# A fused attention and expert kernel on one core: identity transposes ahead of the first products, later casts, stores in pieces, two tiles reordered

## The reference

```python
scores = q @ k.T / sqrt(64)          # block-causal mask, blocks of 64
attn   = exp(scores - max); attn /= attn.sum() + 1e-9
x      = (attn @ v) as [2304, 512]
p      = domain_probs / (sum + 1e-9)               # 4 experts
y      = sum over e of p[:, e] * (relu(x @ w1[e]) @ w2[e])     # 512 -> 1024 -> 512
h      = y @ w_in                                  # 512 -> 1024
solu   = h * softmax(h)
out    = layernorm(solu) * g_ln @ w_out            # 1024 -> 512
```

## Time and profile before

| | |
|---|---|
| median of 3 runs | 1168.68 us (1168.49 to 1169.01) |
| profiled execution, its own time | 1172.1 us |
| its span, first to last instruction | 1170.3 us |
| PE busy | 1140.5 us, 97% |
| DVE, ACT, POOL busy | 55%, 36%, 36% |
| mean granted clock of PE | 0.995 |

### The profile page before, as it was taken

How to read it: one execution, slowest core, us unless ns; L and a number is a source line. 1 busy time by engine, 2 the same in 40 slices (tenths; PEclk the granted TensorE clock), 3 DMA queues, 4 the chain that set the end, 5 groups by cost and what they waited for, 6 DMA issues and landing times.

```text
span 1170.3 us, 16702 instructions
## 1 busy us (share of the span) xinstructions
PE 1140.5 (97%) x6114; PEld 1020.3 (87%) x6114; DVE 645.2 (55%) x1155; ACT 425.8 (36%) x927; POOL 415.7 (36%) x403
## 2 busy tenths in 40 slices
PE   7999998899999999999999999999999999999998
PEld 6999888888989999999999999999999977888886
DVE  7999987554244534333444334452434468667774
ACT  6888876231223311112321112321112344433432
POOL 6898886572434200005400004410002463433320
PEclk8999999999999999999999999999999999999999
DMA  4575765985563313071504052512225100000000
GB/s 140 184 223 177 233 224 182 366 288 207 194 219 117 127 57 132 9 252 55 207 1 189 1 195 85 186 57 103 87 82 198 37 18 10 27 20 27 19 27 36
DMA packets 67477, 146.28 MB, mean 125 GB/s; under 512 B 5968, under 2 KB 34640, under 8 KB 67280
## 3 DMA queue, kind: packets, MB, share of 16 engines
q1 hardware_dynamic: 67408, 145.36, 35.6%
HBM read 114.60 MB, written 30.74 MB: 124 GB/s over the span
## 4 chain that ended last, share of the span: by engine, by line
PE 79%; DVE 5%; POOL 5%; DMA 4%; issue 3%; ACT 2%; SPq 1%; DVEq 0%; POOLq 0%; ACTq 0%
PE s L1700 34%; PE outp L1564 18%; PE s L1564 12%; PE ring L1564 10%; DMA work<-x_rows 2%; PE ring L1575 1%; DVE neg_max L1179 1%; PE ring L1831 1%; POOL x_late L749 1%; ACT pr L894 1%; DVE ptr_l L1186 1%; PE outp L1610 1%; PE outp L1609 1%; DVE k_l L1191 1%; DMA xr<-x_stash 1%
## 5 line engine op out<-in xcount | busy, mean ns | idle before, releaser
L1700 PE MATMUL s<-xr,w1s 128*128 128x384 f32 x2016 | 360.4, 337 | 4.8 <-DVE u L1394 4.3
L1700 PEld LDWEIGHTS s<-xr,w1s 128*128 128x128 f32 x2016 | 351.8, 188 | 9.5 <-DVE u L1394 5.0
L1034 ACT ACTIVATE hid_h<-u 128x384 fp32r<-128x384 f32 x96 | 50.4, 525 | 365.5 <-DVE u L1389 338.7
L708 POOL TENSOR_TENSOR work<-work 128x256 f32<-128x256 f32 x20 | 15.9, 796 | 395.2 <-DMA work<-in_moe_w 269.3
L1344 DVE SCALAR_TENSOR_TENSOR hid_l<-s,hid_h 128x384 fp32r<-128x384 f32 x48 | 26.8, 557 | 124.8 <-ACT hid_h L1030 124.8
L1564 PE MATMUL s<-k_h,qb 128*128 128x288 f32 (+8 forms) x320 | 78.1, 332 | 10.1 <-DVE qb L1262 5.6
L1700 PE MATMUL s<-w1s,yop_h 128*128 128x512 f32 x252 | 85.7, 399 | 1.9 <-POOL yop_l L851 0.7
L1301 DVE TENSOR_TENSOR u<-s,m_b 128x384 f32<-128x384 f32 x24 | 13.4, 558 | 130.0 <-PE s L1700 130.0
L1030 ACT ACTIVATE hid_h<-s 128x384 fp32r<-128x384 f32 x48 | 23.6, 491 | 157.6 <-PE s L1564 154.5
L894 ACT ACTIVATE pr<-s,neg_max 128x576 f32<-128x576 f32 (+2 forms) x144 | 75.6, 533 | 6.8 <-DVE neg_max L1179 6.5
L1564 PE MATMUL outp<-w_h,hid_h 128*128 128x512 f32 x192 | 75.5, 393 | 0.0
(11 more groups left out here) (170 smaller groups left out, 2454.0 us busy)
## 6 DMA issues: line engine op xcount, KB each, us to landing
xr<-x_stash SPq DMA_DIRECT2D x77, 768.0 KB, 6.4
r_sb<-r_scratch SPq DMA_DIRECT2D x16, 576.0 KB, 4.3
x_rows<-x_n SPq DMA_DIRECT2D x32, 288.0 KB, 4.7
work<-x_rows SPq DMA_DIRECT2D x24, 384.0 KB, 6.5
x_stash<-x_tmp SPq DMA_DIRECT2D x12, 768.0 KB, 4.2
work<-in_moe_w SPq DMA_DIRECT2D x32, 256.0 KB, 3.9
stage<-in_moe_w SPq DMA_DIRECT2D x32, 256.0 KB, 4.9
x_stash<-xr SPq DMA_DIRECT2D x1, 5376.0 KB, 21.6
```

What stands on the lines that cost most here:

```text
L708: pool.tensor_tensor(s1, a21, a22, ALU.add).then_inc(w1_sums, 1)
L1034: act.activation(hid[slot][0][:, :], source, ACT.Relu).then_inc(hid_high, 1)
L1700: last = pe.matmul(target, x, y, start=start and i == 0, stop=stop and i == 2, skip_group_check=True)
```

## The change

PE makes 17 transposes of the identity into `ring` as soon as the identity exists, which POOL now makes first. POOL starts on the queries of pair 1 only when DVE has split those of pair 0. DVE makes `key_low(1)` behind all row maxima of pair 0. In the steps 10 to 14 the casts and low parts of x, and the load of its second half, are placed otherwise. In `last_step` the product m2 moves ahead of the last turn. The store of `xr` becomes seven stores, issued behind the store of the last pair's output and the loads that follow it. The casts of rounds 0 and 1 with t = 1 move from the middle of units 2 and 6 to their end. In the last stage, `ln_low_part` of the last tile but one goes ahead of the last tile's variance, and the first half of that tile's output ahead of the last `turn_ln`.

```diff
@@ SP
-            def load_x(sg, t):
+            def load_x(sg, t, parts=(0, 1)):
                 for i in range(2):
                     sp.wait_ge(x_stored[i], 16 * min(PAIRS, DC * (sg + 2)))
                 if sg == 0 and t == 0:
                     sp.wait_ge(w1_ready, 3 * HALF_F)
+                elif parts == (1,):
+                    sp.wait_ge(x_added, 2 * sg + t)
                 elif 2 * sg + t < 3:
                     sp.wait_ge(x_low, NR * (2 * sg + t - 1) + 2)
...
                 if n == 1:
-                    sp.wait_ge(stash_stored, 16)
+                    sp.wait_ge(stash_stored, 16 * NP)
...
                 if p == 9:
                     load_x(0, 0)
+                if p == 12:
+                    load_x(0, 1, (0,))
                 if p + 2 < PAIRS:
                     load_k(p + 2)
                 store_r(p)
                 spread_r(p)
-                if p == 12:
-                    load_x(0, 1)
+                if p == 11:
+                    load_x(0, 1, (1,))
...
-            sp.wait_ge(x_low, 2 * NR)
-            sp.dma_start(x_stash[0, :, :], xr[:, :].bitcast(f32)).then_inc(stash_stored, 16)
+            def stash_first(slots):
+                for i in slots:
+                    at = i * SLOT
+                    sp.dma_start(x_stash[0, :, at:at + SLOT], xr[:, at:at + SLOT].bitcast(f32)).then_inc(stash_stored, 16)
+
             store_x(PAIRS - 1)
-
             sp.wait_ge(w2_ready, 2)
             load2(w2[0, :, :], 2)
             load_x(1, 1)
+            sp.wait_ge(x_low, 2 * NR)
+            stash_first(range(0, 3))
             stash_round(1, 0, 0)
             stash_round(1, 0, 1)
             sp.wait_ge(w2_ready, 4)
             load2(w2[0, :, :], 3)
+            stash_first(range(3, NP))
             stash_round(1, 0, 2)
             stash_round(1, 0, 3)
             load_x(2, 0)
@@ POOL
-            pool.memset(v_nat[:, (KC - 1) * P:KC * P], 0.0).then_inc(tail_clear, 1)
             pool.memset(ident[:, :], 0.0).then_inc(consts_step, 1)
             pool.wait_ge(consts_step, 1)
             pool.affine_select(out=ident[:, :], in_=ident[:, :], compare_op=ALU.not_equal, fill=1.0, base=0,
-                               pattern=[[-1, P]], channel_multiplier=1).then_inc(consts_made, 1)
+                               pattern=[[-1, P]], channel_multiplier=1).then_inc(ident_made, 1)
+            pool.memset(v_nat[:, (KC - 1) * P:KC * P], 0.0).then_inc(tail_clear, 1)
...
-            pool.wait_ge(consts_made, 3)
+            pool.wait_ge(ident_made, 1)
+            pool.wait_ge(tail_clear, 1)
+            pool.wait_ge(first_split, 3)
             split_query(1)
             for p in range(PAIRS):
-                if p == 11:
-                    x_low_part(0, 0, 0)
-                if p == 12:
-                    x_low_part(0, 0, 2)
-                    x_low_part(0, 0, 3)
                 split_values(p)
...
                 if p == 11:
+                    x_low_part(0, 0, 0)
                     x_low_part(0, 0, 1)
                 if p == 12:
                     x_join(0, 1)
                 if p == 13:
+                    x_low_part(0, 0, 2)
+                    x_low_part(0, 0, 3)
                     x_add(0, 1, 0)
                     x_add(0, 1, 1)
+                if p == 14:
                     x_low_part(0, 1, 0)
-                if p == 14:
                     x_low_part(0, 1, 1)
@@ ACT
                 if p in (10, 11):
-                    x_cast(0, 0, 2 * (p - 10))
-                if p in (13, 14):
-                    x_cast(0, 1, 2 * (p - 13))
+                    x_cast(0, 0, p - 10)
+                if p == 14:
+                    x_cast(0, 1, 1)
+
+            def nearly_late(p):
+                if p == 11:
+                    x_cast(0, 0, 2)
+                if p == 14:
+                    x_cast(0, 1, 2)
 
             def late(p):
...
-                if p in (10, 11):
-                    x_cast(0, 0, 2 * (p - 10) + 1)
+                if p == 11:
+                    x_cast(0, 0, 3)
                 if p in (13, 14):
-                    x_cast(0, 1, 2 * (p - 13) + 1)
+                    x_cast(0, 1, 3 * (p - 13))
...
                 high(T452, p, par)
+                nearly_late(p)
                 exp_scores(5, n)
...
-                if e == 0 and sg < 2 and u in (1, 2):
-                    x_cast(sg + 1, u - 1, 0)
-                    x_cast(sg + 1, u - 1, 1)
+                if e == 0 and sg < 2 and u == 1:
+                    x_cast(sg + 1, 0, 0)
+                    x_cast(sg + 1, 0, 1)
...
                 hid_rest(m, "c12", 3, u2[:, :])
+                if e == 0 and sg < 2 and u == 2:
+                    x_cast(sg + 1, 1, 0)
+                    x_cast(sg + 1, 1, 1)
@@ DVE
             max_scores(8, 0)
-            max_scores(7, 0)
+            for b in SCORE_ORDER[1:]:
+                max_scores(b, 0)
             key_low(1, 1)
-            for b in SCORE_ORDER[2:]:
-                max_scores(b, 0)
...
             moments(TT - 1)
+            ln_low_part(TT - 2)
             variance(TT - 1)
             normalise(TT - 1)
-            ln_low_part(TT - 2)
             ln_low_part(TT - 1)
@@ PE
                 turn(T452, p, par)
+                up(0, "m2")
                 turn(T0123, p, par)
                 all_right(p)
-                up(0, "m2")
                 up(0, "m7")
...
-            pe.wait_ge(consts_made, 3)
+            pe.wait_ge(ident_made, 1)
+            for _ in range(WARM_TURNS):          # WARM_TURNS = 17
+                pe.transpose(ring[:, 0:P], ident[:, :], ident[:, :])
+            pe.wait_ge(consts_made, 2)
...
             output(TT - 3, 1)
+            output(TT - 2, 0)
             turn_ln(TT - 1)
-            output(TT - 2, 0)
             output(TT - 2, 1)
```

More of the change, by code:

```diff
@@ L54, in build_program @@
     GROUPS_S = len(SCORE_GROUPS)
+    WARM_TURNS = 17
     def keys(b):
@@ L301, in build_program @@
         first_split = sem("first_split")
+        ident_made = sem("ident_made")
         tail_clear = sem("tail_clear")
@@ L540, in load_x @@
                     sp.wait_ge(x_added, 2 * sg + t)
-                for z, rows in enumerate((x_top, x_bottom)):
+                for z in parts:
+                    rows = x_bottom if z else x_top
                     for h in range(2):
```

## The result

The changed kernel takes 1172.91 us (median of 8 runs, 1171.25 to 1173.74), the kernel before beside it 1168.85. The ratio is 1.0031, 95% interval [1.002, 1.0042]. The forecast was 1160.5 us, faster. By the ratio it is slower by some 3.6 us: the sign is wrong, and the value lies outside the range.

The account below looks back on a forecast made before the run. PE's own products were taken as the bound (busy 1140.5 of 1170.3 us), leaving idle and low-clock time to gain. Terms -4.2 - 3.5 - 4.2 + 5.3 - 1.6 = -8.2 off 1168.7 gave 1160.5 us, range 1154.5 to 1166.0.

Parts of the forecast that it names:

- head: Kernel start through attention step 1: transposes, earlier reciprocals and no fall of the clock save 4.2 us; bounds -1.5 and -5.0.
- attention steps 10 to 15: Waits on queries and `ptr_l` go, two casts add 1.6 us to the path: net -3.5 us; bounds -5.0 and -1.0.
- store of the last pair: End of unit 1: PE's 3.34 us stall and 1.3 us of low clock go, 0.4 kept back: -4.2 us.
- casts at the end of units 2 and 6: Copies stall m2 and operands of units 4 and 8 come late: +5.3 us; bounds +1.2 and +9.
- tail: Last stage: PE's 1.69 us wait for a low part goes: -1.6 us; bounds -1.2 and -1.7.
- what is late next, for which 0.4 us had been kept: After the last pair's store: POOL's `x_join` and low parts run beside DVE's combinations, 0.4 us held back.
- slower rival: Four 768 KB `xr` stores delay rounds 2 and 3, stalling unit 2's casts: +11 us, 1171.5 us; chance 0.07.
- The 4.2 us that the prediction set against the rival: Landing time of the stores of rounds 2 and 3, against the over 12 us at which the slower rival decides.
- PE's first wait on `qb`: Kernel start: a sign of the forecast, that this wait is near 1.5 us.
- The rival that the transposes warm nothing: Head: first products stay at the lower clock, so head is -3.0 and the time 1161.7 us; chance 0.2.
- Alone on the queue it should be faster, so I take 1.5 and not 2.1: Unit 8: a 19.5 us chain of casts, low parts, stores and load makes operands late, +1.5 us.
- the third operand: Next group after the casts: PE needs it 17.4 us from the casts, against a 20.6 us chain: +2.6 us.

Follow-up runs that it names:

- e4: The kernel before with only the head's edits (17 transposes, identity first, later query split, `key_low(1)` behind the maxima): 1166.85 us, 0.9994.
- e8: e1 with attention steps 10 to 15 as before the change on all engines: 1166.07 us, 0.9984.
- e1: The changed kernel with the casts of t = 1 back behind c11 in the middle of units 2 and 6: 1163.0 us, 0.9956.
- e10: The kernel before with only SP's new order: last pair's store ahead, store of `xr` in seven pieces: 1170.34 us, 1.0017.
- e2: The kernel before with only the late casts at the end of units 2 and 6: 1175.97 us, 1.0083.
- e9: The kernel before with only the tail's two lines moved: 1166.35 us, 0.9985.
- e5: The kernel before, unchanged, traced in a second execution: 1167.13 us.
- e13: e10 with the last four pieces of the `xr` store moved behind the stores of rounds 2 and 3: 1173.75 us, 1.0049.
- e6: The changed kernel with the casts of units 2 and 6 one place earlier, between ACT's casts of c22 and c21: 1167.88 us, 1.0001.
- e11: e1 with POOL's join for the next super-group behind low parts 2 and 3 of t = 1: 1161.35 us, 0.9947.
- e12: e1 run again, beside e11: 1163.77 us, 0.9963.
- e7: The changed kernel with POOL's join for the next super-group behind two low parts of t = 1: 1172.2 us, 1.0031.
- e3: The changed kernel without its 17 transposes: 1172.15 us, 1.0036.
- e15: e11 with the store of `xr` as before the change, one store ahead of the last pair's: 1160.24 us, 0.9929.
- e14: e11 with the last four pieces of the `xr` store moved behind the stores of rounds 2 and 3: 1165.96 us, 0.9983.

## Why the prediction was wrong

| term | forecast | measured |
|---|---|---|
| head | -4.2 | -0.7 (e4) |
| attention steps 10 to 15 | -3.5 | -3.3 (e8 against e1) |
| store of the last pair | -4.2 | +2.0 (e10) |
| casts at the end of units 2 and 6 | +5.3 | +8.8 (after against e1), +9.7 (e2) |
| tail | -1.6 | -1.8 (e9) |
| sum | -8.2 | +5.0 to +5.9 |

The measured terms are ratios less 1 (or less the other kernel's ratio), times 1168.5 us. Each is uncertain by 1 to 2.5 us, so their sum does not contradict the 3.6 us of the whole. Nor need they add: the +2.0 of the store was measured with early casts, which wait for stores behind the pieces, and the late casts of after do not. An estimate for its place in after is what separates after from e2 (3.1 and 8.3 thousandths, -6.1 us) less head, steps and tail (-5.8): about nothing.

**The store of the last pair, 6 us off.** The term was the stall of 3.34 us and the 1.3 us of low clock. In e5, e2, e9 and e4 the stall is 0.24 to 0.99 us. In e5 ACT did wait too, 6.24 us for the same rows, and PE hardly felt it: most of this wait was slack. The prediction took one execution, itself 3.4 us above the median, and took "the same differences off the median". Where the profiled execution is that far above the median, what it has beyond the others is what a change can't give back. Besides, the pieces are not free. Of what is late next, for which 0.4 us had been kept, PE has the 1.21 us on DVE, in e10 and in after. The slower rival was right that the stores of rounds 2 and 3 are held up by the four pieces, 9.8 us where 4.1 is usual (e10, e5), and right that 12 us decide: in after they had landed when the casts came, so this rival did not come about there. It did in e10, whose casts come earlier, and the whole of the edit costs 2.0 us there. The 4.2 us that the prediction set against the rival is a median over twelve stores of the whole span, and these stand behind 3 MB. The sign of the whole is not explained by this rival.

**The head, 3.5 us off.** By most of its own steps it was right: the transposes fit (1.52 to 5.16), no clock of 0.5 near 16, the gap ahead of step 0 1.30 us, step 1 at 25.84. Only PE's first wait on `qb` is 0.54 us and not 1.5. What failed is the other side of the difference, the head of before. The 1.4 us between steps 0 and 1 were the low spell of one execution: in the five others that have the old head (e5, e2, e9, e10, e13) these steps are 10.7 to 10.8 us apart, after has 10.86, and nothing is gained. Mark 0 is at 15.52, 17.19, 17.36, 15.34 and 17.79 in them, so there the gain is 0.4 to 2.8 us, with 17.33 no rare value. Of this, 0.7 us reach the end in e4. Where the rest goes stays open.

The rival that the transposes warm nothing is refuted (0.73 against 1.16 us for the same products of block 7). The Trainium skill, TensorE: Matmul & The Clock Gate, "Part 4: PE-mode transpose", says that transpose mode does not count as busy for the clock; in after, e6, e11 and e12 the 17 fp32 transposes were all that PE had done when it came to the first product at the higher level, so these traces do not agree. In the other seven with transposes that product still ran at the lower level. Whether the time gains by them is not shown: 1.0031 with them, 1.0036 without.

**The casts, some 4 us off.** The copy of m1 costs 0.97 us twice, forecast 1.1. The wait in unit 2 that was to go, 1.00 in the trace of before, is 0.61 in e1 and gone in after. Unit 4: 3.12 us of waits where e1 has 1.87, and 1.7 us of clock, together 2.9; forecast 2.6. The failed step is unit 8, "Alone on the queue it should be faster, so I take 1.5 and not 2.1". The length of the chain was right in sum: 19.5 us were worked out and 19.4 passed from the casts (305.89) to PE's start on the first load (325.29). Its parts were not, which is luck: 8.4 us to ACT's second cast where 6.6 were forecast, 4.2 from there to the load's issue where 6.6 were, as the load doesn't wait for the last store to land, and 6.8 for the load where 6.3 were. What was wrong is when PE needs it. The prediction asked after the third operand, 17.4 us behind the casts, because the one wait in the trace before stood there. When all seven loads shift together, the first is the late one, and PE wants it at 321.55, 15.7 us behind the casts. 19.4 less 15.7 is the 3.7 us seen. It was the first because SP's written order has all four stores of the round chain ahead of all seven loads, so even the operands of round 1 wait for round 3. The clock that a wait of this size costs, 1.7 us, had been put in the bound and not in the value. By the traces the term is 1.9 less 0.6, and 2.9 and 5.4 (3.74 and 1.7): 9.6 us. This, too, is one execution of after: in the other kernels with late casts the first wait at unit 8 is 3.38 us (e7), 2.10 (e2) and 1.56 (e3, with the clock left up). The size of the term rests on the times of e1 and e2, not on the trace.

**Steps and tail: right.** Waits on the queries and on `ptr_l` went. Those on the reciprocals grew by 1.4 us (1.6 forecast), but not where the forecast had them: behind steps 11 and 14 they are 0.34 and 0.91 us, before nothing and 0.70 us, and most of the growth is at marks 10, 13 and 14. Two waits are new that the prediction didn't name, 0.62 us on `k_l` and 0.91 us on POOL's low part of x. So part of the agreement of the steps' term is luck. The last low part lies under twelve products.

**The chances.** The store and a third of the head rested on accidents of one execution, so they were wrong together, and the casts fell the same way. A chance of 0.88 for faster left no room for that. That the trace itself might be unusual, with its time 3.4 us above the median in plain view, was no rival, and should have been the first.

## What to carry to other kernels

Before a stall is priced as a gain, ask whether it is there in a usual execution: a profile above the median holds accidents, and they are no income. When a producer is moved later, follow its chain to the first consumer of the whole batch of transfers, not to the one that happens to wait today, and count the queue's written order in between. A large store is best put where nothing behind it is needed soon. In this kernel splitting it did not help: whatever stood behind the pieces came later.

## What the runs showed of the hardware

- A wait of PE of 2.57 or 3.74 us was followed by 3.4 us at 1.2 GHz (after, at 257.4 and 325.6). The level did not depend on a long wait alone. In e10 and e15 such a spell of 3.4 us began at 197.1 and 187.9, behind pairs of waits of 1.01 and 0.91 us and of 0.91 and 0.92 us; after has a pair of 0.91 and 0.91 us at 187.57 and 189.77 and no spell. In e14 a wait of 1.71 and one of 1.99 us left the clock at 1.0, and in e3 one of 2.21 us at 14.76 did, where before lost it behind 2.19 us at 14.74.
- Seventeen fp32 transposes of the identity from 1.52 us on brought the higher clock for block 7's scores in all 11 kernels that have them (0.62 to 0.81 us for two products of 512 columns, against 1.06 to 1.22 in the seven without).
- Four pieces of 768 KB (issued from 222.48) and then 1152 KB of stores: 9.8 us from the issue of the latter until the cast that waits for them. In e5, where the one store of 5376 KB (issued at 198.18, 20.0 us to landing) was over, the same 1152 KB took 4.1 us.
- Two executions of the same program differ in where they lose time: the turn of the reciprocals of step 0 came at 17.33 and at 15.52 us.
